# Scores and new state of the linear attention in two PSUM banks and in two steps of the feed-forward loop

## The reference

```python
# 1 linear attention: batch 4, heads 8, sequence 768, head_dim 48
for t in range(S):
    cur = einsum('bhd,bhe->bhde', u * k[t], v[t])
    y[t] = einsum('bhd,bhde->bhe', r[t], state + cur)
    state = w[..., None] * state + einsum('bhd,bhe->bhde', k[t], v[t])
# 2 feed-forward: (3072, 384) @ (384, 2048), leaky with a slope per column, @ (2048, 384)
h = x @ w_in
x = (maximum(h, 0) + alpha * minimum(h, 0)) @ w_out
# 3 routed layer: 8 experts, 384 tokens each, given out greedily by the largest logit
#   out[mask_e] = maximum(x[mask_e] @ w1[e], 0) @ w2[e]
```

## Time and profile before

| | us |
|---|---|
| median of 3 runs | 832.35 |
| lowest and highest | 830.99, 833.05 |
| the profiled execution | 832.35 |
| its span | 830.5 |
| TensorE busy in the span | 779.7 (94%) |
| VectorE busy | 514.6 (62%) |
| GpSimd busy | 476.9 (57%) |
| ScalarE busy | 210.0 (25%) |
| mean granted TensorE clock | 0.971 |

### The profile page before, as it was taken

How to read it: one execution, slowest core, us unless ns; L and a number is a source line. 1 busy time by engine, 2 the same in 40 slices (tenths; PEclk the granted TensorE clock), 3 DMA queues, 4 the chain that set the end, 5 groups by cost and what they waited for, 6 DMA issues and landing times.

```text
span 830.5 us, 15950 instructions
## 1 busy us (share of the span) xinstructions
PE 779.7 (94%) x6316; PEld 657.4 (79%) x6324; DVE 514.6 (62%) x1040; ACT 210.0 (25%) x432; POOL 476.9 (57%) x469
## 2 busy tenths in 40 slices
PE   5779899999999999999999999947999999999996
PEld 3567777888788878887888888725889989989996
DVE  7876566666666666666666333477777777776221
ACT  1223221111211121112111211104244344353451
POOL 6679884655465546554654343207475775675881
PEclk8989999999999999999999999958999999999999
DMA  7775421222222222222000000015514505418401
GB/s 211 181 192 140 128 78 58 67 68 67 68 67 69 67 67 68 67 67 68 29 11 11 10 21 9 10 39 181 181 38 174 206 15 200 165 46 276 143 20 38
DMA packets 46649, 75.17 MB, mean 91 GB/s; under 512 B 6256, under 2 KB 31984, under 8 KB 46576
## 3 DMA queue, kind: packets, MB, share of 16 engines
q1 hardware_dynamic: 38176, 56.66, 21.9%
q10 hardware_dynamic: 5328, 8.06, 3.4%
q0 software_dynamic: 3072, 9.44, 3.1%
HBM read 64.71 MB, written 9.44 MB: 89 GB/s over the span
## 4 chain that ended last, share of the span: by engine, by line
PE 74%; POOL 9%; DVE 8%; issue 4%; DMA 2%; ACT 2%; POOLq 0%; ACTq 0%; SPq 0%; DVEq 0%
PE bank L1141 21%; PE bank L1142 19%; PE bank L1143 19%; POOL gl L448 4%; PE bank L1190 3%; PE bank L1156 2%; PE bank L1246 2%; PE bank L1375 2%; PE bank L1173 2%; DVE grid L1037 2%; PE bank L1318 2%; DMA x2T<-w_out 1%; POOL wout_l L388 1%; POOL win_l L388 1%; DVE grid L1035 1%
## 5 line engine op out<-in xcount | busy, mean ns | idle before, releaser
L448 POOL TENSOR_TENSOR gl<-g,gh 128x512 fp32r<-128x512 f32 x96 | 128.6, 1340 | 204.7 <-ACT gh L574 204.7
L574 ACT CAST gh<-g 128x512 fp32r<-128x512 f32 x96 | 59.6, 621 | 358.8 <-PE bank L1143 307.8
L885 DVE TENSOR_SCALAR q<-bank,alpha_sb 128x512 f32<-128x512 f32 x96 | 72.0, 750 | 125.9 <-PE bank L1143 125.5
L1141 PE MATMUL bank<-gh,wout_h 128*128 128x512 f32 x288 | 118.8, 413 | 3.2 <-POOL gl L448 2.7
L1141 PE MATMUL bank<-xTh,win_h 128*128 128x512 f32 x288 | 113.3, 393 | 0.3 <-DVE xTl L778 0.3
L1142 PE MATMUL bank<-gl,wout_h 128*128 128x512 f32 x288 | 112.8, 392 | 0.0
L1143 PE MATMUL bank<-gh,wout_l 128*128 128x512 f32 x288 | 112.8, 392 | 0.0
L1142 PE MATMUL bank<-xTl,win_h 128*128 128x512 f32 x288 | 112.5, 391 | 0.0
L1143 PE MATMUL bank<-xTh,win_l 128*128 128x512 f32 x288 | 112.3, 390 | 0.0
L512 POOL TENSOR_TENSOR w1l<-raw,w1h 128x384 fp32r<-128x384 f32 x64 | 65.4, 1021 | 28.3 <-ACT w2h L631 28.1
L888 DVE SCALAR_TENSOR_TENSOR g<-bank,q 128x512 f32<-128x512 f32 x96 | 66.4, 692 | 7.6 <-POOL gl L448 4.5
(11 more groups left out here) (175 smaller groups left out, 1500.8 us busy)
## 6 DMA issues: line engine op xcount, KB each, us to landing
raw<-w SPq DMA_DIRECT2D x32, 768.0 KB
kt<-kT SPq DMA_DIRECT2D x48, 96.0 KB, 2.7
rt<-rT SPq DMA_DIRECT2D x48, 96.0 KB, 2.8
vs<-v SPq DMA_DIRECT2D x48, 96.0 KB, 2.9
vn<-v SPq DMA_DIRECT2D x24, 192.0 KB, 3.0
x2rows<-x2n SPq DMA_DIRECT2D x24, 192.0 KB, 1.9
kn<-kN SPq DMA_DIRECT2D x20, 192.0 KB, 2.4
rn<-rN SPq DMA_DIRECT2D x20, 192.0 KB, 2.6
```

The costliest lines, as they stand in the source:

```text
L448: nc.gpsimd.tensor_tensor(gl[:, f % 2], g[:, f % 2], gh[:, f % 2].bitcast(F32), ALU.subtract).then_inc(gl_ready, 1)
L574: nc.scalar.copy(gh[:, f % 2], g[:, f % 2]).then_inc(gh_ready, 1)
L885: nc.vector.tensor_scalar(q[:, f % 2], h, 0.0, alpha_sb[:, f:f + 1], ALU.min, ALU.mult).then_inc(q_ready, 1)
L1141: nc.tensor.matmul(o, a_h, b_h, start=first, stop=False)
```

## The change

Half 0 of the scores and of the new state now goes to bank 5, half 1 to bank 6 (chunks 1 to 5). Scores lie on partitions 0 to 63 of bank 5 and 64 to 127 of bank 6, new states on the others. `new_state` is issued one step later, at f % 4 = 1. `scores` waits for `s_updated` of the batch before (which `new_state` used to wait for), and `new_state` waits for both masks of its own batch. `mask` waits for the scores of its half only.

```diff
--- before.py
+++ after.py
@@ -234,10 +234,10 @@
             return banks[0] if first(c) else banks[7]
 
         def score_bank(c, b, j):
-            return banks[(1 if b == 1 else 5) + j] if first(c) else banks[5]
+            return banks[1 + j] if first(c) and b == 1 else banks[5 + j]
 
         def state_bank(c, b, j):
-            return banks[(1 if b % 2 else 3) + j] if first(c) else banks[6]
+            return banks[(1 if b % 2 else 3) + j] if first(c) else banks[5 + j]
 
         def weights(c, b):
             if not first(c) or b % 2 == 0:
@@ -740,7 +740,7 @@
 
             def mask(c, b):
                 for j in range(2):
-                    dve.wait_ge(scores_done, 8 * c + 2 * b + (j + 1 if first(c) else 2))
+                    dve.wait_ge(scores_done, 8 * c + 2 * b + j + 1)
                     rows = halves(j)
                     nc.vector.tensor_tensor(weights(c, b)[rows, j], score_bank(c, b, j)[rows].rearrange("p (h t) -> p h t", h=H),
                                             before[rows, rows].unsqueeze(1).to_broadcast([HALF, H, HT]), ALU.mult).then_inc(masked, 1)
@@ -1147,8 +1147,10 @@
                 if first(c):
                     if b >= 2:
                         pe.wait_ge(masked, 2 if b == 2 else 6)
+                elif isinstance(c, int) and c == 1 and b == 0:
+                    pe.wait_ge(masked, 8)
                 else:
-                    pe.wait_ge(masked, 8 * c + 2 * b)
+                    pe.wait_ge(s_updated, 8 * c + 2 * b)
                 wait(pe, x2n_ready, B * (c - 2) + b + OUT_PRE)
                 wait(pe, logits_ready, B * (c - 2) + b + OUT_PRE)
                 for h in range(H):
@@ -1163,10 +1165,8 @@
                 pe.wait_ge(kpad_ready, B * c + b + 1)
                 if first(c) and b >= 2:
                     pe.wait_ge(s_updated, 2 * b - 2)
-                elif first(c):
-                    pe.wait_ge(masked, 2 * b + 2)
-                elif c > 1 or b > 0:
-                    pe.wait_ge(s_updated, 8 * c + 2 * b)
+                else:
+                    pe.wait_ge(masked, 8 * c + 2 * b + 2)
                 for h in range(H):
                     cols = slice(h * D, (h + 1) * D)
                     for j in range(2):
@@ -1254,13 +1254,7 @@
                     if isinstance(i, int) and i == 0 and f == 0:
                         hidden(i, 1)
                     if attention:
-                        if f % 4 == 0:
-                            scores(i + 1, f // 4)
-                            new_state(i + 1, f // 4)
-                        if f % 4 == 2:
-                            attend(i + 1, f // 4)
-                        if f % 4 == 3:
-                            turn(i + 1, f // 4)
+                        (scores, new_state, attend, turn)[f % 4](i + 1, f // 4)
                     if output and f % 4 == 2:
                         output_tile(i - 1, f // 4)
                     if f >= 2:
```

## The result

The changed kernel takes 837.48 us (median of 7 runs, 835.70 to 839.78), the kernel before 831.53 us (7 runs, 830.99 to 833.05, the three of the prediction's base among them). The ratio is 1.0074, with a 95% interval of 1.0056 to 1.0092: 6.0 us slower, or 4.7 to 7.6. The changed kernel was timed once more later, beside other runs of the kernel before: 838.62 against 832.66 us, ratio 1.0068 (1.0054 to 1.0082). Its profiled execution was one of the longer ones: 840.72 us, span 838.9.

A forecast was written before the change was run, and what follows sets the result against it. Chunks 1 to 4 were taken as bound by TensorE's own stream, chunk 0 as leaving it room. 4.96 - 0.96 + 1.02 = +5.02 us on 832.35 gave 837.4 us, range 833.8 to 839.8.

The forecast's parts named there:

- The seams: Chunks 1 to 4, TensorE: splitting scores from new_state adds an entry and exit per batch, 16 x 0.31 = +4.96 us.
- Attend's wait: Batch 0 of chunks 1 to 4: attend no longer waits for VectorE's state update, 4 x 0.24 = -0.96 us.
- The added waits: New_state waiting for both masks and scores for the previous batch's state update: all covered, nothing charged.
- Chunk 0: Batch 3's new_state, hidden before in the wait ahead of back(10), becomes exposed: +1.02 us; batches 0 to 2 cost nothing.
- The free seam: Rival: new_state's extra seam costs nothing in chunks 1 to 4, giving 832.2 us; chance 0.12, shared with half price.
- The banks: Rival: two banks make the halves of scores and new_state faster, -9.8 us, giving 822.6; chance 0.05.
- The clock: Rival: idle ahead of back(10) in chunk 0 lowers TensorE's clock, 1.7 us more, giving 839.1; chance 0.13 for losing more.
- the upper bound: New_state entered from a big product: its added seam was bounded between 0 and 0.31 us per batch; 0.31 was taken.

The follow-up runs named there:

- without the move: Kernel before with new_state of batches 1 to 3, chunks 1 to 4, inside the same step's back: 836.51 us against 832.66, ratio 1.0041.
- the filled kernel: Changed kernel with five extra bf16 products ahead of back(2), back(6) and back(10) of chunk 0: 837.92 us against 831.96 for the kernel before.
- Joining islands: Kernel before with earlier VectorE updates, and scores and new_state of batches 1 to 3 right behind turn in chunks 1 to 4: 831.33 us against 832.66.
- chunk 0 left alone: Kernel before with new_state one step later in the loops of chunks 1 to 4 only: 836.84 us against 831.96, ratio 1.0068.

## Why the prediction was right

*Direction and size.* 837.4 us was forecast and 837.48 measured; but the base of the forecast was 832.35, the median of three runs, and over seven runs the kernel before took 831.53. The forecast loss was 5.0 us and the measured one is 6.0 (4.7 to 7.6). The sum was 1 us short, and part of the agreement of the two totals is luck. The direction and the size of the loss are not: the second comparison gives 6.0 again, and the terms are found one by one.

*The seams* (4.96 forecast). The mechanism holds: it is shown with the move alone, without the move, and with the banks alone as the control. The term was undersized: 0.36 instead of 0.31 for a batch. The forecast had the entry (0.32), the 0.10 by which scores are left later (1.08 instead of 0.98) and the exit (0.34), less two pitches. Two parts were missing. New_state, entered from a big product, takes 0.85 us to the next start, while behind scores it takes 0.81. And the products behind a seam are a little slower: 16 pitches behind one (as from 156.96 to 160.62) take 3.65 us on average instead of 3.63, and a second seam slows a second row of them. The prediction took new_state's 0.81 from a row where it stands behind scores, and priced a seam by its edges alone; a price from mark to mark, attend to attend, has all of it. With 16 x 0.36 = 5.8 the sum fits the chunks: 5.8 - 0.96 = 4.8, measured 4.92.

*Attend's wait* (-0.96 forecast). Batch 0 loses 0.13 us from the last big product ahead of scores to attend (135.88 to 142.54 before, 138.26 to 145.05 now), the other batches 0.36, so 0.23 came back per chunk. Removed by itself it is worth 0.96 in the trace, which the timed runs are too coarse to confirm.

*The added waits* (nothing forecast). At batch 0 the masks are done 0.45 us ahead of new_state, forecast 0.43, and in all 16 places of the trace scores and new_state start 0.32 us behind the last big product, so no wait shows.

*Chunk 0* (+1.02 forecast). New_state exposed at batch 3 costs 1.06 to 1.10 us in the three traces without the clock's fall there. It is sharp because the stretch from back(10) to the wait for gl(15) is steady: 18.40 to 18.44 us in the six traces with chunk 0's order of before, 19.47 to 19.51 in those three. What batches 0 to 2 cost, forecast as nothing, goes under in scatter: from the start of the loop to back(10) it is 70.8 to 72.7 us in the same six traces and 72.0 to 72.3 in the four with the new order. With 4.92 for chunks 1 to 4, the 1.06 makes 5.98 us, well inside the 4.7 to 7.6 of the runs; that it meets the 6.0 of the medians so closely is chance.

*The rivals.* The free seam is refuted by every trace that has a second seam: 0.35 or 0.36 each. The banks are refuted as a gain by a kernel that has only them. The clock came as described, in some executions: 1.65 us where it fell at back(10) (forecast 1.7), nothing at back(2). How often it falls is not settled; the filled kernel gives no sign that it carries the median. The length of one idle doesn't decide it either, as the last section lists.

*The rule on tiling modes.* The Trainium skill, page "TensorEngine Tiling (Array Packing)", Key Properties, says that changing the tiling mode drains TensorE. That was right to speak for the upper bound. The trace agrees on the entry: 0.32 us into the half-array groups, 0.23 into the full-array transpositions. It agrees less on the exit, since the transpositions are left with 0.32 to the second big product too, where by the rule no mode changes. So a part of the seam, about 0.1 us of the 0.36, is not explained by that rule, and no run here separates what TensorE does in the rest: the price is shown, not its inner cause. By Gotcha 1 of the same page of the Trainium skill different row tiles cannot access one bank at once. This shows as no cost in time here: scores run into new_state after 0.98 us and new_state into the next product after 0.81 or 0.82, with two banks as with one.

## What to carry to other kernels

Where TensorE is the bound, as in chunks 1 to 4 here, small groups between big products are cheapest in few, long islands: each extra island cost 0.36 us, almost half of what the new_state group itself takes (0.81), though not one matmul is added. Spreading such groups to even out the steps pays only if a wait of more than that goes away for it; here one of 0.24 us did, once in four batches. Look first whether the order of the engine that is waited for can be changed instead, as with VectorE's update, which gave the same 0.24 us per chunk in the trace without any new seam. Joining islands is no sure gain: through the transpositions it saved 0.03 us a place. And a group that stands where TensorE would wait for another engine anyway is free there, and need not be one step later: new_state at batch 3 of chunk 0 cost 1.06 us.

## What the runs showed of the hardware

- The two groups of half-array float32 products, scores and new_state, take the same time with their two halves in one PSUM bank as in two: 1.15 and 0.89 us in both, as the profile gives them (ratio of the kernels 1.0001, 0.9988 to 1.0015).
- A seam has a tail: the 16 pitches behind it take 3.65 us against 3.63 in undisturbed rows (0.2283 and 0.2267 each; changed kernel, chunks 1 to 4). The excess lies in the first five, 0.231, 0.236, 0.228, 0.233 and 0.231 us on average. It is there behind full-array transpositions too.
- Leaving three full-array transpositions for half-array products takes 0.42 us from the first start, leaving them for full-array products 0.24. They are entered from a big product after 0.23 us, half-array groups after 0.32.
- Two idles of 1.99 and 2.00 us ahead of back(2) were followed by the clock of 1.2 GHz in both traces of the changed kernel, 0.9 to 1.0 us after work had begun again (68.34 and 69.22; 69.17 and 70.18). An idle of 1.50 was followed by it at once in one trace, while 1.32 and 1.47 at the same place in two others were not, nor was 1.76 ahead of back(6) in the trace of the later step alone. In the trace with chunk 0 left alone it fell behind 1.03 and 0.76 us; behind 0.96 and 0.76 at that place before, it did not. What decides it is not shown.
